# A fused convolution and two-layer kernel on one core: 64-row products of two chunks on the two row halves, g's high part on ScalarE, and a cosine without squaring

## The chip, the core and the metric

The kernel runs on one core of a Trainium2 chip. The core has five engines that run beside each other, each through its own queue in order: TensorE (PE in the profile, its weight loads PEld), VectorE (DVE), ScalarE (ACT), GpSimd (POOL), and SyncE (SP), which issues transfers. They tell each other of finished work by semaphores: an instruction can wait for one and raise one. TensorE multiplies weights of 128 rows with, here, mostly 512 columns of data and adds the results up in PSUM; the data and the weights lie in SBUF. The metric is the time of one execution on the device, in microseconds (us); less is better.

## The reference

```python
# x: 4 x 4096 x 192; weight: 8 x 7
w = softmax(weight)                                       # 7 taps of each of 8 groups of 24 channels
x = causal_conv(x, w).reshape(16384, 192)                 # every channel with the taps of its group
h = x @ moe_w_in;  g = h * np.cos(h);  x = g @ moe_w_out  # 192 -> 2048 -> 192
h = np.maximum(x @ moe2_w_in, 0.0)
out = h * h @ moe2_w_out                                  # 192 -> 2048 -> 192
```

All arrays are f32, and so is the result.

## The kernel before

**Tiles and turns.** The 16384 rows are 32 tiles of 512 tokens; on the chip a tile lies with channels or features in the 128 partitions and tokens along the columns. A *turn* works on four tiles at once: X transposes tile i+1's rows and runs its convolution, A is the first layer (the cosine) of tile i, B the second (the squared relu) of tile i-1, and Y transposes tile i-2's result and stores it. A layer's 2048 features are 16 chunks of 128, taken as 8 *pairs*. Turns -1 to 2 and 31 to 33 are written out; the 28 between are a hardware loop.

**The order within a turn** is a table by hand, `SLOTS`: 18 slots, numbered from 0, as A0 A1 B0 A2 X B1 A3 B2 A4 B3 A5 Y A6 B4 A7 B5 B6 B7. Every engine walks through this table in a `body` of its own, and each does its part of a slot s, or of an earlier one (`turn.earlier(s, n)` is the slot n before s, which at a turn's start is in the turn before). The first tile has another table, `FIRST_SLOTS`.

**Products in parts.** Each operand of a product is kept as a high part rounded to fp32r (`_hi`) and what is left of it (`_lo`). 192 channels are 128 and a *side* of 64. `up(slot)` makes h for the two chunks of a pair; each chunk takes five products of 128 rows: the side's low weights (`up_side_lo`), low weights by high x, high weights by low x, the side's high weights (`up_side_hi`), high by high. The side's x tile, `xin_side`, has its high part in one half of the 128 rows and its low part in the other, and the side's weights stand in both halves. `down(slot)` takes five products of a chunk from `g_hi` and `g_lo` into `y`. TensorE does in slot s `up` of s and then `down` of slot s-3 (`LAG = 3`), if that is an A or a B; so slots 7 and 14, three behind X and Y, have no `down`. h has two buffers in PSUM (`HB = 2`), g and its parts four (`RING = 4`).

**What makes g.** For an A slot: ScalarE reads h into g, scaled by 1/(2 pi) (line 434); VectorE takes the distance to the nearest whole number (`fraction`, lines 529 and 531) into `w`; ScalarE takes the sine of it times pi and squares that (`half_cosine`, lines 444 and 446); VectorE multiplies (`times_cosine`, line 537); GpSimd rounds a copy of g to `g_hi` (line 631); VectorE subtracts that from g for `g_lo` (`low_part`, line 543), for which `down` waits (line 338). For a B slot ScalarE does the relu and the square (lines 436, 438), then GpSimd and VectorE as before. `half_cosine`, `times_cosine`, the copy to `g_hi` and `low_part` are done in slot s for slot s-1; in VectorE's walk `fraction` of s comes first, then `times_cosine`, the taps of the convolution (`TAP_SLOTS`), and `low_part`. At a turn's end stand the splits of x into its parts: the convolution's in slots 15 and 16 (lines 479, 480, 576, 578), layer 1's result in slot 0 (lines 459, 460, and on VectorE `split_layer2`, lines 586 to 594).

**The weights of layer 2** are loaded and split during the first tile, in three rounds in slots 9, 12 and 15 (`LATE_SLOTS`): ScalarE makes the high parts (`late_hi`), GpSimd the low parts (`late_lo_part`) between its copies to `g_hi`, and SyncE then reloads the staging buffer.

## Time and profile before

| | us |
|---|---|
| median of 3 runs | 2639.35 |
| the runs | 2638.49 to 2639.89 |
| profiled execution, first to last instruction | 2636.2 |

A busy share says how long an engine had an instruction in work. TensorE's is modelled: a 512-column product is shown with 0.39 us, yet in a dense stretch the next begins 0.227 us later. So the pace is read from the starts in the timeline, and what an engine waited for from the waits. The turns repeat, so that one of them, here that of 1322 to 1402 us, stands for the loop.

### The profile page before, as it was taken

The numbers are of one execution on the slowest core, as the hardware profiler recorded it, in microseconds if no ns is written. First come the engines' busy times: TensorE is split into PE (matmuls) and PEld (weight loads), VectorE is DVE, ScalarE is ACT, GpSimd is POOL, SyncE is SP. The second block draws the span as 40 slices with busy tenths as digits, with TensorE's granted clock in tenths as the row PEclk, the third lists the DMA queues.
The fourth block names the chain that finished last, engine by engine and source line by source line (L and its number), as shares of the span: only waits on it lengthen the run. The fifth ranks groups of instructions, "written<-read, shape, count | busy, mean of one in ns | idle before, by whom it ended". The sixth has DMA issues, their size and how long they took to land. (4 is left out here: it accounts for less than half of the span.)

```text
span 2636.2 us, 30240 instructions
## 1 busy us (share of the span) xinstructions
PE 2467.1 (94%) x10880; PEld 2003.5 (76%) x10880; DVE 2127.3 (81%) x2060; ACT 1484.8 (56%) x1549; POOL 682.4 (26%) x523
## 2 busy tenths in 40 slices
PE   5799999999999999999999999999999999999998
PEld 4577787777877777777777777778777778777787
DVE  7888888888888887888888888888888888888863
ACT  4455565655555555555555565555656556565554
POOL 2322222222222222222222222222222222222221
PEclk9899999999999999999999999999999999999999
DMA  3100000000000000000000000000000000000000
GB/s 101 36 1 13 13 6 12 12 6 12 12 6 12 6 12 12 12 6 12 6 12 12 6 12 12 6 12 12 6 12 6 12 12 6 12 12 6 6 7 13
DMA packets 39457, 32.89 MB, mean 12 GB/s; under 512 B 1676, under 2 KB 38668, under 8 KB 39180
## 3 DMA queue, kind: packets, MB, share of 16 engines
q1 hardware_dynamic: 39260, 32.61, 4.2%
q8 instruction: 13, 0.21, 0.0%
q14 instruction: 8, 0.07, 0.0%
q10 hardware_dynamic: 176, 0.00, 0.0%
HBM read 20.03 MB, written 12.58 MB: 12 GB/s over the span
## 5 line engine op out<-in xcount | busy, mean ns | idle before, releaser
L631 POOL TENSOR_SCALAR g_hi<-g 128x1024 fp32r<-128x1024 f32 x512 | 658.6, 1297 | 1920.6 <-DVE g L537 1612.2
L543 DVE TENSOR_TENSOR g_lo<-g,g_hi 128x1024 fp32r<-128x1024 f32 x512 | 744.4, 1459 | 167.7 <-POOL g_hi L631 162.0
L444 ACT ACTIVATE w<-w 128x1024 f32<-128x1024 f32 x256 | 271.5, 1061 | 751.2 <-DVE w L531 751.2
L537 DVE SCALAR_TENSOR_TENSOR g<-w,g 128x1024 f32<-128x1024 f32 x256 | 315.7, 1233 | 241.6 <-ACT w L446 239.0
L434 ACT ACTIVATE g<-h 128x1024 f32<-128x1024 f32 x256 | 261.3, 1021 | 268.1 <-PE h L322 268.1
L338 PE MATMUL y_A<-g_hi,dn_lo_A 128*128 128x512 f32 x512 | 222.0, 434 | 125.3 <-DVE g_lo L543 124.6
L531 DVE TENSOR_TENSOR w<-w,g 128x1024 f32<-128x1024 f32 x256 | 313.7, 1225 | 8.8
L436 ACT ACTIVATE g<-h 128x1024 f32<-128x1024 f32 x256 | 259.4, 1013 | 34.8 <-PE h L322 34.6
L438 ACT ACTIVATE g<-g 128x1024 f32<-128x1024 f32 x256 | 271.9, 1062 | 8.1
L446 ACT ACTIVATE w<-w 128x1024 f32<-128x1024 f32 x256 | 271.6, 1061 | 8.1
L570 DVE SCALAR_TENSOR_TENSOR conv_side<-xt_side,taps,conv_side 64x512 f32<-64x512 f32 x192 | 251.3, 1309 | 6.2
L338 PEld LDWEIGHTS y_A<-g_hi,dn_lo_A 128*128 128x128 f32 x512 | 99.1, 194 | 181.8 <-DVE g_lo L543 161.7
L318 PE MATMUL h<-x_side_A,up_side_lo_A 128*128 128x512 f32 x512 | 201.9, 394 | 30.9 <-DVE x_side_A L578 30.9
L529 DVE TENSOR_SCALAR w<-g 128x1024 f32<-128x1024 f32 x256 | 177.8, 695 | 54.0 <-ACT g L434 52.4
L339 PE MATMUL y_A<-g_hi,dn_side_A 128*128 128x512 f32 x512 | 208.2, 407 | 0.0
L340 PE MATMUL y_A<-g_hi,dn_hi_A 128*128 128x512 f32 x512 | 207.8, 406 | 0.0
L341 PE MATMUL y_A<-g_lo,dn_side_A 128*128 128x512 f32 x512 | 206.9, 404 | 0.0
L342 PE MATMUL y_A<-g_lo,dn_hi_A 128*128 128x512 f32 x512 | 206.3, 403 | 0.0
L318 PE MATMUL h<-x_side_B,up_side_lo_B 128*128 128x512 f32 x512 | 201.1, 393 | 2.1 <-ACT g L436 1.1
L338 PE MATMUL y_B<-g_hi,dn_lo_B 128*128 128x512 f32 x512 | 199.6, 390 | 1.4 <-DVE g_lo L543 1.3
L319 PE MATMUL h<-x_hi_B,up_lo_B 128*128 128x512 f32 x512 | 200.5, 392 | 0.0
L320 PE MATMUL h<-x_lo_B,up_hi_B 128*128 128x512 f32 x512 | 200.1, 391 | 0.0
(90 smaller groups left out, 4669.3 us busy)
## 6 DMA issues: line engine op xcount, KB each, us to landing
rows_in<-x SPq DMA_DIRECT2D x32, 384.0 KB, 3.3
out<-late SPq DMA_DIRECT2D x32, 384.0 KB, 2.6
late<-w_out SPq DMA_DIRECT2D x2, 1536.0 KB, 10.2
g<-w_in SPq DMA_DIRECT2D x1, 1024.0 KB, 5.2
g<-w_in SPq DMA_DIRECT2D x2, 512.0 KB, 8.1
late<-w_in SPq DMA_DIRECT2D x2, 512.0 KB, 4.5
late<-w_in SPq DMA_DIRECT2D x4, 256.0 KB, 5.7
taps<-weight ACTq DMA_DIRECT2D x4, 0.7 KB
```

The lines of the kernel that those rows point to most:

```text
L318: pe.matmul(dst, up_side_lo[kind][:, f], xin_side[kind][:, :], start=True, stop=False)
L338: pe.matmul(y[kind][:, 0, :], dn_lo[kind][:, c, :], hi, start=a, stop=False)
L434: act.activation(g[:, r, :, :], src, ACT.Copy, scale=1.0 / TWO_PI).then_inc(taken["A"], 1)
L436: act.activation(g[:, r, :, :], src, ACT.Relu).then_inc(taken["B"], 1)
L438: act.activation(g[:, r, :, :], g[:, r, :, :], ACT.Square).then_inc(relu_sq, 1)
L444: act.activation(v, v, ACT.Sin, scale=math.pi).then_inc(sine, 1)
L446: act.activation(v, v, ACT.Square, scale=math.sqrt(2.0)).then_inc(sine_sq, 1)
L531: dve.tensor_tensor(v, v, u, ALU.subtract).then_inc(frac, 1)
L537: dve.scalar_tensor_tensor(out=u, in0=v, scalar=1.0, in1=u, op0=ALU.subtract, op1=ALU.mult).then_inc(g_made, 1)
L543: dve.tensor_tensor(g_lo[:, r, :, :], g[:, r, :, :], g_hi[:, r, :, :].bitcast(F32), ALU.subtract).then_inc(lo_made[kind], 1)
L570: dve.scalar_tensor_tensor(out=conv_side[side, :], in0=xt_side[side, k:k + TOK], scalar=taps[side, 1, k:k + 1], in1=conv_side[side, :], op ...
L631: return pool.tensor_scalar(dst, src, 1.0, 0.0, ALU.mult, ALU.add)
```

## The change

The products (TensorE). A chunk's `up` has four products of 128 rows: the side's, low by high, high by low, high by high. The side's weights are now one tensor, `up_side`, with the high part in one half of the rows and, in the other, the low part; what is missing, high weights by the side's high x, is one product of 64 rows for each chunk. For the even chunk it is done on the one row half, for the odd chunk on the other, as the last two products of the pair. For this the even chunks' weights stand a second time (`up_even`) and the side's high x a second time (`x_odd`).

g's high part. ScalarE makes it (`high_part`), in slot s for slot s-2, behind its reading of slot s. VectorE's `low_part` is now that of slot s-2 as well. GpSimd's loop is gone; it keeps the low parts of the weights, one behind the other. `LAG` is unchanged.

The cosine. `fraction` rounds u + 1/4 and keeps w = round(u + 1/4) - u; ScalarE takes one sine with a scale and a bias of a quarter turn (`turned_cosine`), always ahead of its reading of the slot; VectorE multiplies, and does so ahead of the next `fraction`.

```diff
-                    pe.matmul(dst, up_side_lo[kind][:, f], xin_side[kind][:, :], start=True, stop=False)
+                    pe.matmul(dst, up_side[kind][:, f], xin_side[kind][:, :], start=True, stop=False)
                     pe.matmul(dst, up_lo[kind][:, f], xin_hi[kind][:, :], start=False, stop=False)
                     pe.matmul(dst, up_hi[kind][:, f], xin_lo[kind][:, :], start=False, stop=False)
-                    pe.matmul(dst, up_side_hi[kind][:, f], xin_side[kind][:, :], start=False, stop=False)
-                    mm = pe.matmul(dst, up_hi[kind][:, f], xin_hi[kind][:, :], start=False, stop=True)
+                    pe.matmul(dst, up_hi[kind][:, f], xin_hi[kind][:, :], start=False, stop=False)
+                even, odd = hi_rows[kind], lo_rows[kind]
+                f = slice((p * PAIR + 1) * P, (p * PAIR + 2) * P)
+                pe.matmul(h[:, s % HB, 0, :], up_even[even, p, :], xin_side[kind][even, :], start=False, stop=True)
+                mm = pe.matmul(h[:, s % HB, 1, :], up_side[kind][odd, f], xin_odd[odd, :], start=False, stop=True)
...
-            def half_cosine(turn, p, back):
+            def turned_cosine(turn, p, back):
                 v = w[:, p % WB, :, :]
                 act.wait_ge(frac, turn.count("A", p, back))
-                act.activation(v, v, ACT.Sin, scale=math.pi).then_inc(sine, 1)
-                act.wait_ge(sine, turn.count("A", p, back))
-                act.activation(v, v, ACT.Square, scale=math.sqrt(2.0)).then_inc(sine_sq, 1)
+                act.activation(v, v, ACT.Sin, bias=quarter[:, 0:1], scale=-TURN).then_inc(cosine, 1)
+
+            def high_part(turn, e, kind, p, back):
+                r = turn.ring(e, back) % RING
+                before = Turn(turn.i - back, TILES, turn.i8 - NP * back)
+                freed = before.before(before.pairs, before.ring(e), RING)
+                if freed:
+                    act.wait_ge(used[freed[0]], freed[1])
+                act.wait_ge({"A": g_made, "B": relu_sq}[kind], turn.count(kind, p, back))
+                act.activation(g_hi[:, r, :, :], g[:, r, :, :], ACT.Copy).then_inc(hi_made[kind], 1)
...
                     if turn.runs(kind):
                         read_h(turn, s, kind, p)
-                    if cosine and kind == "A" and turn.runs("A"):
-                        half_cosine(turn, q, back)
+                    e, back, made, q = turn.earlier(s, 2)
+                    if made in "AB" and turn.runs(made, back):
+                        high_part(turn, e, made, q, back)
...
                         act.activation(xin_side["A"][P - SIDE:P, :], conv_side[P - SIDE:P, :], ACT.Copy)
+                        act.activation(xin_odd[0:SIDE, :], conv_side[P - SIDE:P, :], ACT.Copy)
...
-                dve.tensor_scalar(v, u, ROUND, ROUND, ALU.add, ALU.subtract).then_inc(whole, 1)
+                dve.tensor_scalar(v, u, 0.25, ROUND, ALU.add, ALU.add).then_inc(whole, 1)
                 dve.wait_ge(whole, turn.count("A", p))
-                dve.tensor_tensor(v, v, u, ALU.subtract).then_inc(frac, 1)
+                dve.scalar_tensor_tensor(out=v, in0=v, scalar=ROUND, in1=u, op0=ALU.subtract,
+                                         op1=ALU.subtract).then_inc(frac, 1)
...
+                dve.tensor_copy(xin_odd[SIDE:P, :], y_side[low, :])
                 dve.tensor_copy(xin_side["B"][low, :], y_side[low, :]).then_inc(x2_step, 1)
...
+                    if last == "A" and turn.runs("A", back):
+                        times_cosine(turn, r, q, back)
                     if kind == "A" and turn.runs("A"):
                         fraction(turn, turn.ring(s) % RING, p)
-                    if last == "A" and turn.runs("A", back):
-                        times_cosine(turn, r, q, back)
...
-                    if last in "AB" and turn.runs(last, back):
-                        low_part(turn, r, last, q, back)
+                    e, back, made, q = turn.earlier(s, 2)
+                    if made in "AB" and turn.runs(made, back):
+                        low_part(turn, turn.ring(e, back) % RING, made, q, back)
```

Where the instructions stand. On TensorE the `up` of one pair, A, before:

```order
L318 MATMUL h<-x_side_A,up_side_lo_A 128x512
L319 MATMUL h<-x_hi_A,up_lo_A 128x512
L320 MATMUL h<-x_lo_A,up_hi_A 128x512
L321 MATMUL h<-x_side_A,up_side_hi_A 128x512
L322 MATMUL h<-x_hi_A,up_hi_A 128x512
L318 MATMUL h<-x_side_A,up_side_lo_A 128x512
L319 MATMUL h<-x_hi_A,up_lo_A 128x512
L320 MATMUL h<-x_lo_A,up_hi_A 128x512
L321 MATMUL h<-x_side_A,up_side_hi_A 128x512
L322 MATMUL h<-x_hi_A,up_hi_A 128x512
```

and after:

```order
L330 MATMUL h<-x_side_A,up_side_A 128x512
L331 MATMUL h<-x_hi_A,up_lo_A 128x512
L332 MATMUL h<-x_lo_A,up_hi_A 128x512
L333 MATMUL h<-x_hi_A,up_hi_A 128x512
L330 MATMUL h<-x_side_A,up_side_A 128x512
L331 MATMUL h<-x_hi_A,up_lo_A 128x512
L332 MATMUL h<-x_lo_A,up_hi_A 128x512
L333 MATMUL h<-x_hi_A,up_hi_A 128x512
L336 MATMUL h<-x_side_A,up_even 128x512
L337 MATMUL h<-x_odd,up_side_A 128x512
```

Still ten products; the last two, lines 336 and 337, are those on half the rows.

On ScalarE, in the loop, slots 7 and 8 (B2 and A4), before; line 434 and 436 read an A and a B, `w<-w` is the sine and its square, `g<-g` the relu's square:

```order
L444 ACTIVATE w<-w 128x1024
L446 ACTIVATE w<-w 128x1024
L414 REGISTER_ALU
L436 ACTIVATE g<-h 128x1024
L438 ACTIVATE g<-g 128x1024
L414 REGISTER_ALU
L434 ACTIVATE g<-h 128x1024
```

and after, where line 456 reads B2, line 454 A4, and line 474 is the copy to `g_hi`:

```order
L464 ACTIVATE w<-w,quarter 128x1024
L434 REGISTER_ALU
L456 ACTIVATE g<-h 128x1024
L458 ACTIVATE g<-g 128x1024
L474 ACTIVATE g_hi<-g 128x1024
L434 REGISTER_ALU
L454 ACTIVATE g<-h 128x1024
L474 ACTIVATE g_hi<-g 128x1024
```

The squared sine is gone, and behind each reading stands the copy of the pair two slots back.

On VectorE, in the loop, slots 8 and 9 (A4 and B3), before; lines 529 and 531 are the fraction of A4, 537 the product with the cosine, 568 and 570 a tap of the convolution:

```order
L529 TENSOR_SCALAR w<-g 128x1024
L531 TENSOR_TENSOR w<-w,g 128x1024
L542 REGISTER_ALU
L543 TENSOR_TENSOR g_lo<-g,g_hi 128x1024
L537 SCALAR_TENSOR_TENSOR g<-w,g 128x1024
L567 REGISTER_ALU
L568 SCALAR_TENSOR_TENSOR conv<-xt,taps,conv 128x512
L570 SCALAR_TENSOR_TENSOR conv_side<-xt_side,taps,conv_side 64x512
L543 TENSOR_TENSOR g_lo<-g,g_hi 128x1024
```

and after:

```order
L559 TENSOR_SCALAR w<-g 128x1024
L561 SCALAR_TENSOR_TENSOR w<-w,g 128x1024
L573 TENSOR_TENSOR g_lo<-g,g_hi 128x1024
L568 TENSOR_TENSOR g<-w,g 128x1024
L597 REGISTER_ALU
L598 SCALAR_TENSOR_TENSOR conv<-xt,taps,conv 128x512
L600 SCALAR_TENSOR_TENSOR conv_side<-xt_side,taps,conv_side 64x512
L572 REGISTER_ALU
L573 TENSOR_TENSOR g_lo<-g,g_hi 128x1024
```

The rows have the same order, but the first `g_lo` is that of A3 after the change, where it was B2's before, and the second that of B2, where it was A4's.

## Rows read from the trace of the kernel before

**Rows 1.** The page, part 1: each engine's busy us, share of the span, instructions.
```profile
PE 2467.1 (94%) x10880; PEld 2003.5 (76%) x10880; DVE 2127.3 (81%) x2060; ACT 1484.8 (56%) x1549; POOL 682.4 (26%) x523
```

**Rows 2.** The waits: who waited for whom, us in total, times, longest.
```profile
DVE g L537 <- ACT w L446: 239.0, 188, 2.2
...
PEld y_A L338 <- DVE g_lo L543: 161.7, 114, 6.8
```

**Rows 3.** The edge copy, line 552: times, ns min/median/max, first and last start.
```profile
L552 DVEq FUSED_REGOPS  x28: 75/75/75, 285.0 to 2451.9; - x28
```

**Rows 4.** Timeline: start us, us, engine line op, tile; TensorE, `up` to `down`.
```profile
1326.54 0.39 PE L322 MATMUL h<-x_hi_B,up_hi_B 128*128 128x512 f32 x1
1326.77 0.39 PE L338 MATMUL y_B<-g_hi,dn_lo_B 128*128 128x512 f32 x1
```

**Rows 5.** Timeline, weight loads of X's transposes.
```profile
1321.33 0.14 PEld L354 LDWEIGHTS h<-ident,rows_in 128*128 128x128 f32 x1
1321.44 0.14 PEld L353 LDWEIGHTS h<-ident,rows_in 128*128 128x128 f32 x1
```

**Rows 6.** Timeline, TensorE and VectorE around a wait; brackets: idle before, and releaser.
```profile
1368.21 0.39 PE L322 MATMUL h<-x_hi_B,up_hi_B 128*128 128x512 f32 x1
1368.48 1.95 DVE L543 TENSOR_TENSOR g_lo<-g,g_hi 128x1024 fp32r<-128x1024 f32 x1
...
1370.48 0.50 PE L338 MATMUL y_A<-g_hi,dn_lo_A 128*128 128x512 f32 x1 [1.89 <-DVE g_lo L543]
...
1370.82 0.40 PE L339 MATMUL y_A<-g_hi,dn_side_A 128*128 128x512 f32 x1
```

**Rows 7.** Timeline, ScalarE: a B slot's pair, and two copies in the first tile.
```profile
45.76 1.04 ACT L403 ACTIVATE up_hi_B<-late 128x1024 fp32r<-128x1024 f32 x1
46.71 1.04 ACT L404 ACTIVATE up_side_hi_B<-late 128x1024 fp32r<-128x1024 f32 x1
...
1326.97 1.03 ACT L436 ACTIVATE g<-h 128x1024 f32<-128x1024 f32 x1 [0.26 <-PE h L322]
1328.03 1.06 ACT L438 ACTIVATE g<-g 128x1024 f32<-128x1024 f32 x1
```

**Rows 8.** Timeline, an A slot's reading on ScalarE and VectorE behind it; two VectorE steps.
```profile
1334.17 1.23 DVE L531 TENSOR_TENSOR w<-w,g 128x1024 f32<-128x1024 f32 x1
1335.32 1.22 DVE L543 TENSOR_TENSOR g_lo<-g,g_hi 128x1024 fp32r<-128x1024 f32 x1
...
1390.30 1.03 ACT L434 ACTIVATE g<-h 128x1024 f32<-128x1024 f32 x1 [3.58 <-PE h L322]
1391.36 0.69 DVE L529 TENSOR_SCALAR w<-g 128x1024 f32<-128x1024 f32 x1 [1.47 <-ACT g L434]
1392.09 1.23 DVE L531 TENSOR_TENSOR w<-w,g 128x1024 f32<-128x1024 f32 x1
```

**Rows 9.** Timeline, VectorE at a turn's start: y's split, then A0's fraction.
```profile
1384.20 0.68 DVE L586 TENSOR_TENSOR y_side<-y_A,y_side 64x512 f32<-64x512 f32 x1
1384.91 0.57 DVE L589 CAST x_side_B<-y_side 64x512 fp32r<-64x512 f32 x1
1385.40 0.67 DVE L591 TENSOR_TENSOR x_lo_B<-y_A,x_hi_B 128x512 fp32r<-128x512 f32 x1
1386.09 0.69 DVE L594 TENSOR_TENSOR x_side_B<-y_side,x_side_B 64x512 fp32r<-64x512 f32 x1
1386.80 0.69 DVE L529 TENSOR_SCALAR w<-g 128x1024 f32<-128x1024 f32 x1
```

**Rows 10.** Line 543, `g_lo`: times, ns min/median/max, first and last start.
```profile
L543 DVE TENSOR_TENSOR g_lo<-g,g_hi x512: 1210/1225/3382, 40.6 to 2625.9; 128x1024 fp32r<-128x1024 f32 x171
```

**Rows 11.** Busy us by engine in 8 us; behind POOL's the granted clock.
```profile
1448.00:1456.00 8.00, 6.15 (x20) 4.58 (x20) 6.85 (x7) 3.60 (x5) 1.43 (x2) 0.79 0.00 0
```

**Rows 12.** Timeline, ScalarE: the first tile's first reading of A, and the next's.
```profile
31.25 1.03 ACT L434 ACTIVATE g<-h 128x1024 f32<-128x1024 f32 x1 [6.62 <-PE h L322]
...
101.95 1.03 ACT L434 ACTIVATE g<-h 128x1024 f32<-128x1024 f32 x1 [1.08 <-PE h L322]
```

More of the change, by code:

```diff
@@ L59 @@
 ROUND = 1.5 * 2.0 ** 23
+TURN = 13176794.0 * 2.0 ** -21
+QUARTER = 13176794.0 * 2.0 ** -23
 def at(t):
@@ L162, in tile_program @@
         xin_side = {k: sb(f"x_side_{k}", [P, TOK], F32R) for k in "AB"}
+        xin_odd = sb("x_odd", [P, TOK], F32R)
+        low, high = slice(0, SIDE), slice(SIDE, P)
+        hi_rows, lo_rows = {"A": high, "B": low}, {"A": low, "B": high}
         g = sb("g", [P, RING, PAIR, TOK])
@@ L207, in tile_program @@
         taken = {k: sem(f"taken_{k}") for k in "ABXY"}
-        sine = sem("sine")
-        sine_sq = sem("sine_sq")
+        cosine = sem("cosine")
         relu_sq = sem("relu_sq")
@@ L281, in _ @@
                 sp.wait_ge(late_lo, 2 * half + 2)
+                if half:
+                    sp.wait_ge(even_made, half)
                 cols = slice(half * HALF, (half + 1) * HALF)
@@ L450, in body @@
                     _, back, last, q = turn.earlier(s, 1)
-                    cosine = last == "A" and turn.runs("A", back)
-                    if cosine and not (kind == "A" and turn.runs("A")):
-                        half_cosine(turn, q, back)
+                    if last == "A" and turn.runs("A", back):
+                        turned_cosine(turn, q, back)
                     if s == 0 and turn.runs("A", 1):
@@ L603, in body @@
                         split_layer2(turn)
+                    if last == "A" and turn.runs("A", back):
+                        times_cosine(turn, r, q, back)
                     if kind == "A" and turn.runs("A"):
                         fraction(turn, turn.ring(s) % RING, p)
-                    if last == "A" and turn.runs("A", back):
-                        times_cosine(turn, r, q, back)
                     if turn.runs("X") and s == taps_at[0]:
@@ L647, in _ @@
             pool.wait_ge(wi_hi, 1)
-            pool.tensor_tensor(up_side_lo["A"][:, :], stage_in[:, F:2 * F],
-                               up_side_hi["A"][:, :].bitcast(F32), ALU.subtract).then_inc(wi_lo, 1)
-            def body(turn):
-                for s, (kind, p) in enumerate(turn.slots()):
-                    e, back, last, q = turn.earlier(s, 1)
-                    if last in "AB" and turn.runs(last, back):
-                        r = turn.ring(e, back) % RING
-                        before = Turn(turn.i - back, TILES, turn.i8 - NP * back)
-                        freed = before.before(before.pairs, before.ring(e), RING)
-                        if freed:
-                            pool.wait_ge(used[freed[0]], freed[1])
-                        made = {"A": g_made, "B": relu_sq}[last]
-                        pool.wait_ge(made, turn.count(last, q, back))
-                        round_hi(g_hi[:, r, :, :], g[:, r, :, :]).then_inc(hi_made[last], 1)
-                    if turn.peeled and turn.i == 0 and s in LATE_SLOTS:
-                        late_lo_part(1 + LATE_SLOTS.index(s))
-            turns(pool, body)
+            split = up_side["A"][hi_rows["A"], :]
+            pool.tensor_tensor(split, stage_in[hi_rows["A"], F:2 * F], split.bitcast(F32),
+                               ALU.subtract).then_inc(wi_lo, 1)
+            for n in range(1, 1 + len(LATE_SLOTS)):
+                late_lo_part(n)
 def kernel(x, weight, moe_w_in, moe_w_out, moe2_w_in, moe2_w_out):
```

41 lines of the change are left out of this document (23 added, 18 removed).

## The prediction

> **What bounds the kernel now.** The first view is busy time by engine [rows 1]: TensorE (PE) 94%, VectorE 81%, ScalarE 56%, GpSimd 26%. The reader would take TensorE for the bound. The list of waits corrects that [rows 2]: TensorE's largest wait is for `g_lo`, VectorE's last step of a pair, 161.7 us in 114 times; and VectorE itself waits 239.0 us for ScalarE's square. Next, how long is a turn (18 slots, 16 pairs)? The conv's edge copy stands once in a turn; in the loop it stands 28 times, from 285.0 to 2451.9 us, so a turn takes 80.26 us [rows 3]. Then the pace of TensorE: one 512-column product starts 0.227 us after the other [rows 4]. A pair has 20 of them, 4.53 us; 16 pairs are 72.5 us; X and Y I put at 0.9 and 1.0 us, from 0.11 for each of their transposes [rows 5], so 74.4 us are streams and 5.8 us of each turn are waits. One of them is in the timeline [rows 6]: the `up` of a slot is out at 1368.44, `g_lo` ends at 1370.43, TensorE goes on at 1370.48. So at several places of a turn VectorE sets the end; a prediction needs the chain of hand-overs, not the sum of products.
>
> **Part 1, fewer product times.** The side's high part of two chunks is now one product on the lower and one on the upper 64 rows. If the two run beside each other, `up` has 9 product times instead of 10: 2.04 us instead of 2.27, a slot (U + D = `up` + `down`) 4.31 instead of 4.53. No row has a product on half the rows. The lower end of the two's cost is 0.227, since each streams 512 columns and the row has that pace; nothing can be gained below it. The upper end is 2 x 0.227 = 0.454, one after the other. I take 0.227, for the weights need not hold it up: loads for the transposes follow each other in 0.11 us [rows 5], two in 0.22. Saved by itself: 16 x 0.227 = 3.6 us a turn, 109 us in 30 turns.
>
> The Trainium skill is of two minds here. "TensorE: Matmul & The Clock Gate", Part 3, has products on different row groups run concurrently; that agrees with the lower end, and no row here shows it. "TensorEngine Tiling (Array Packing)", Key Properties, says that changing the tiling mode drains TensorE, and each pair would change it twice. That speaks against this change, is a rival below, and no row shows it either.
>
> **Part 2, GpSimd's copy goes to ScalarE, one slot later.** Gone are 512 GpSimd copies. With them goes a slowing of VectorE: `g_lo` has a median of 1225 ns but a longest of 3382 ns [rows 10], and 1.95 us where the copy ran beside it [rows 6]. That is relief on VectorE, hidden wherever the next part decides. Added on ScalarE are 512 copies SBUF to SBUF, 1.04 us each, 0.95 apart from the next [rows 7]; removed are 256 squares of about the same length. ScalarE was busy 1484.8 / 32 = 46.4 us a tile [rows 1]; it gets 16 x 1.04 and loses 8 x 1.06, so some 55 of 80 us, below the bound as a sum. But its order matters. The copy of pair s-2 stands behind the reading of slot s, which waits for `up` of slot s. VectorE's `g_lo` of s-2 stands behind the fraction of slot s, which waits for that reading too. And `down` of s-2 is the `down` of slot s+1, since LAG is still 3. Before, `g_lo` of s-1 was made in slot s, and nothing tied these.
>
> So there is a new chain. Let f be the end of the stream of `up` in slot s, and L the time from f to the `down` that it lets go:
> - A slot: ScalarE starts 0.20 after f [rows 4, 7], reads 1.03, hand-over 0.03, the rounding and its hand-over 0.73, then the second step, behind which `g_lo` starts 1.15 later and takes 1.22 [rows 8], then 0.05 to TensorE [rows 6]. L_A = 4.41.
> - B slot: 0.20, relu to square 1.06, square to copy 0.95, copy 1.04 [rows 7], 0.03, `g_lo` 1.22, 0.05. L_B = 4.55.
> After a pause the first product takes 0.34 instead of 0.227 to the next [rows 6]: 0.11 more. So from one `down` start d to that two slots on, an A slot between them gives 4.31 + 4.41 + 0.11 = 8.83, a B slot 8.97, against 8.62 of pure products where both slots are whole. It bites most where a slot has little for TensorE: X and Y (about 1 us instead of `up`) and slots 7 and 14, which have no `down` (their pair three slots back is X or Y). In slot 8 TensorE has only 2.04 us of `up` after slot 7's, but `down` must wait 4.55: a pause of 2.5 us where there was none.
>
> **Part 3, the turn's end.** The conv split has one more 64x512 copy on ScalarE (under the 1.04 of the wide one; I take 0.6), y's split one more on VectorE (0.49). VectorE does slot 17's `g_lo`, then y's split, then A0's fraction, and only then the `g_lo` of slot 16, wanted in slot 1. From f17: 0.20+1.06+0.95+1.04+0.03 = 3.28 to `g_lo`, 1.15 to y's split, 0.71+0.49+0.49+0.69+0.71 for it, where the 0.49 stands twice for the added copy [rows 9], 0.73+1.15 for the fraction, 1.22 and 0.05, 0.11 restart: 10.78. ScalarE's extra copy is covered by slot 16's `up`, for whose end the next reading waits; the cover is thin, and without it the copy costs its 0.6.
>
> **Part 4, the cosine.** One sine with a bias instead of sine and square: on ScalarE 1.06 us less of a pair; on VectorE the same three steps in other forms, so nothing. The 1.09 us that VectorE idled for the square are gone, but they lay in the old chain. `times_cosine` now stands before the next fraction; the sine ends 4.3 us after f, just when slot s+1's `up` is out, so it hides.
>
> **The sum of a turn.** Take the longest way through the 18 slots from `down` of slot 15 to the next one: two plain slots and the end of the turn (4.31+4.31+10.78 = 19.40) to slot 1; plain, 4.31, to slot 2; through A in slot 3, 8.83, to 4; through B in 5, 8.97, to 6; through B in 7, 8.97, to 8; plain, 4.31, to 9; through A in 10, 12 and 14, 3 x 8.83, to 15. Sum 81.28 us. Of this TensorE's U + D stands in it ten times, so the saving counts 10 x 0.227 and not 16 x.
>
> To it comes the clock. Behind a pause of about 1.9 us the granted clock fell in some turns: 0.79 over 8 us in one turn [rows 11], the lower of the levels 1.2 and 2.4 GHz for a part of it, after TensorE had paused; 8 x 0.21 = 1.7 us of TensorE's time. Now two pauses a turn have about 2.5 us and one 1.8. I take one fall a turn, a third of it on the path: 0.5 us (ends 0 and 3.4). A turn: 81.8 against 80.26, +1.5 us.
>
> **The whole.** 30 turns x 1.5 = +46 us. The first tile: from the first reading of A to the next tile's took 70.7 us [rows 12], because GpSimd had the late weights' low parts and the copies in one queue; now the copies leave that queue, and about 57 us remain (VectorE 4.2 us a pair and the taps, then the last weights' load), while the start has two more copies on ScalarE, some 1.7 us: -12 us (ends -20 and +3). The last tile, products alone: -2 us. So 2636.2 + 46 - 12 - 2 = 2668; outside the span lie 2639.35 - 2636.2 = 3.2 us, so 2671 us against the median of 2639.35, 1.2% slower. An error of 0.1 us in each of the seven hand-overs would be 0.7 us a turn, 21 us.
>
> **The rivals.**
> - Faster: the hand-overs have more slack than I give them (readings or `g_lo` start earlier in the turn than the walk says), and TensorE's stream decides. Then each turn has 16 x 4.31 + 1.9 = 70.9 us and pauses like the old 5.8: 76.7, 3.6 less, 2639 - 107 = 2530; half of that 2585. For it: VectorE's relief is large. Against: the queues' order is fixed, and L rests on rows. It decides from where L falls below 4.2. Chance 0.20.
> - The halves don't overlap (the change doesn't do what it says): 0.454 a pair of products, 10 x 0.227 = 2.27 a turn, +68: 2739. Chance 0.12.
> - Each switch between whole and half rows empties the array. A product shows 0.39 us but paces 0.227 [rows 4], so emptying costs 0.16, twice a pair 0.33; 10 x 0.33 x 30 = +99: 2770. Chance 0.08. (This is the Tiling page's rule above; without that page the price stands.)
> - The clock falls at both long pauses and all of it is on the path: 3.4 instead of 0.5 a turn, +87: 2758. Chance 0.10.
>
> **How the numbers follow.** The forecast, 2671 with its own range of 2640 to 2705, has 0.50. A difference of 0.2%, 5 us, is what a measurement can tell: below 2634 lies the faster rival and a small part of the forecast's lower side, 0.22; within it 0.05; above 0.73. The range goes down to 2560, which takes the nearer half of the faster rival, and up to 2762; left out are the other half (0.10) and the emptying array (0.08).
>
> **What would show it.** In the changed kernel's trace: a turn of 81 to 82 us by the edge copy; waits of TensorE for `g_lo` of both A and B, in sum 9 to 11 us a turn; pauses of about 2.4 us in slots 8 and 15 and 1.7 in slot 1; the two half products starting within some 0.02 us of each other, or else 0.227 apart; `g_lo` near 1.22 in all cases, no 1.95. The forecast is wrong if TensorE's sum of waits stays at 5 us a turn, or if a slot's `g_lo` is made well before `up` of the slot behind it is out.

## The result

| | before | after |
|---|---|---|
| median of the runs on the same chip, us | 2639.11 | 2889.8 |
| the runs, us | 2638.49 to 2639.89 | 2887.75 to 2892.18 |
| profiled execution, us | 2636.2 | 2887.7 |
| a turn by the edge copy, us | 80.26 | 87.12 |
| mean granted clock | 0.985 | 0.963 |

The changed kernel is slower: the ratio of the times is 1.095, interval 1.0935 to 1.0966. The sign was forecast; the size was not, and 2889.8 us lies outside the range of 2560 to 2762.

The page's first part, against [rows 1]:

```profile
PE 2615.2 (91%) x10880; PEld 1921.7 (67%) x10880; DVE 1881.8 (65%) x2093; ACT 1772.4 (61%) x1840; POOL 25.1 (1%) x11
```

The waits (who waited for whom: us in total, times, longest), against [rows 2]:

```profile
PEld h L336 <- issue: 181.0, 512, 0.7
PEld y_A L353 <- DVE g_lo L573: 171.6, 189, 6.3
PEld y_B L353 <- DVE g_lo L573: 142.1, 122, 4.7
...
DVE g L568 <- ACT w L464: 42.7, 35, 1.2
```

The edge copy, now line 582, against [rows 3]:

```profile
L582 DVEq FUSED_REGOPS  x28: 75/75/75, 298.9 to 2651.1; - x28
```

TensorE has 10880 products as before, but 2615 busy us instead of 2467. Its waits for VectorE are now for `g_lo` of A and of B, 171.6 + 142.1 us. VectorE's wait for ScalarE's cosine fell from 239.0 to 42.7 us, and GpSimd is idle: what the change wanted of these two engines it got. A new wait is TensorE's largest, that of the first half product's weights for "issue" (time in which the profile shows nothing that it waited for), once in each of the 512 `up`s. A turn takes (2651.1 - 298.9) / 27 = 87.12 us.

**Where the 251.5 us of the span went.** The 27 turns between the first and the last edge copy: 27 x 6.86 = 185.2. Before the first edge copy: 298.9 - 285.0 = 13.9. Behind the last one: 236.6 instead of 184.3, so 52.3. The two ends together are a quarter of the loss.

**The pair of half products.** TensorE in the timeline of the changed kernel, the end of an `up` of an A and the start of the `down` behind it (start us, us, engine line op, tile, rows*columns of the weights, rows x columns of the data):

```profile
1438.44 0.39 PE L333 MATMUL h<-x_hi_A,up_hi_A 128*128 128x512 f32 x1
1438.76 0.49 PE L336 MATMUL h<-x_side_A,up_even 64*128 64x512 f32 x1
...
1438.76 0.49 PE L337 MATMUL h<-x_odd,up_side_A 64*128 64x512 f32 x1
...
1439.18 0.50 PE L353 MATMUL y_A<-g_hi,dn_lo_A 128*128 128x512 f32 x1
...
1439.52 0.40 PE L354 MATMUL y_A<-g_hi,dn_side_A 128*128 128x512 f32 x1
```

The two halves (lines 336 and 337, `64*128`) start at the same moment. But the first starts 0.32 us behind the whole product ahead of it, the next whole product 0.42 behind them, and the one after that 0.34, where 0.227 is the pace [rows 4]. Beyond one product that is 0.09 + 0.20 + 0.11 = 0.40 us. The pair of halves costs 0.63, two whole products cost 0.454: the change made `up` longer, and a slot takes 4.73 us instead of 4.53. (Of these 0.20 us 0.18 are in the distances just named; the products right behind are a few ns further apart too.)

**The chain of hand-overs.** The same turn from the end of slot 7's `up` to slot 8's `down`, on all engines; in brackets the idle time before an instruction and what ended it:

```profile
1443.48 0.50 PE L337 MATMUL h<-x_odd,up_side_B 64*128 64x512 f32 x1
...
1444.03 1.03 ACT L456 ACTIVATE g<-h 128x1024 f32<-128x1024 f32 x1 [0.53 <-PE h L337]
...
1445.08 1.06 ACT L458 ACTIVATE g<-g 128x1024 f32<-128x1024 f32 x1
...
1446.05 1.04 ACT L474 ACTIVATE g_hi<-g 128x1024 fp32r<-128x1024 f32 x1
...
1447.12 1.23 DVE L573 TENSOR_TENSOR g_lo<-g,g_hi 128x1024 fp32r<-128x1024 f32 x1 [0.93 <-ACT g_hi L474]
...
1448.40 0.50 PE L353 MATMUL y_B<-g_hi,dn_lo_B 128*128 128x512 f32 x1 [1.95 <-DVE g_lo L573]
```

`up` of slot 7 (a B), reading, square, copy to `g_hi`, `g_lo`, `down`: each waits for the one above it, and TensorE stands still for 1.95 us although slot 8's `up` was long out. It is the chain of Part 2, link by link: from the start of the reading, at 1444.03, to the `down` it takes 4.37 us, where the prediction had 1.06 + 0.95 + 1.04 + 0.03 + 1.22 + 0.05 = 4.35. From the `down` of slot 6, at 1439.18, to that of slot 8, at 1448.40, it is 9.22 us, for which the walk had 8.97.

**The clock.** Busy us by engine in stretches of 4 us around this pause; behind POOL's the granted clock:

```profile
1444.00:1448.00 4.00, 2.45 (x10) 1.52 (x10) 3.04 (x4) 3.94 (x5) 0.00 (x0) 1.00 0.00 0
1448.00:1452.00 4.00, 3.60 (x10) 2.84 (x11) 3.88 (x5) 2.10 (x2) 0.00 (x0) 0.67 0.00 0
1452.00:1456.00 4.00, 4.00 (x16) 2.81 (x15) 2.07 (x3) 1.08 (x2) 0.00 (x0) 0.90 0.00 0
```

The granted clock is full ahead of the pause, and then 0.67 and 0.90 in the next two stretches: TensorE ran at the lower of its two levels for a part of them, with 0.43 us between products. The pause in slot 15 of this turn (1.78 us) is followed by a stretch at 0.64. From the `down` of slot 8 to that of 9 it took 6.38 us, from 15 to 16 6.34, where a plain slot takes 4.73 to 4.78: 1.6 us each, and nothing lay beside it. Not every turn has both: of the 54 pauses in slots 8 and 15 of the 27 turns, 41 were followed by such a long slot, 2.4 us a turn in the mean.

### The profile page after: what moved, and what is told of

It is laid out like the page before. It is cut to its first block, busy times and chain, and to the rows that moved or that the text cites. A ratio compares the mean times of both kernels' runs of the same rounds, so it can differ in the third digit from the quotient of the medians.

```text
span 2887.7 us, 29490 instructions
## 1 busy us (share of the span) xinstructions
PE 2615.2 (91%) x10880; PEld 1921.7 (67%) x10880; DVE 1881.8 (65%) x2093; ACT 1772.4 (61%) x1840; POOL 25.1 (1%) x11
## 4 chain that ended last, share of the span: by engine, by line
PE 66%; DVE 18%; ACT 9%; issue 5%; DMA 0%; ACTq 0%; DVEq 0%; SPq 0%
DVE g_lo L573 7%; PE h L330 6%; PE h L331 6%; PE h L332 6%; PE h L333 6%; PE h L336 6%; PE y_A L353 5%; PE y_B L353 5%; DVE w L561 4%; ACT g L454 3%; PE y_B L356 3%; PE y_B L357 3%; PE y_B L355 3%; PE y_B L354 3%; PE y_A L357 3%
## 5 line engine op out<-in xcount | busy, mean ns | idle before, releaser
L573 DVE TENSOR_TENSOR g_lo<-g,g_hi 128x1024 fp32r<-128x1024 f32 x512 | 630.4, 1232 | 582.5 <-ACT g_hi L474 581.4
L474 ACT ACTIVATE g_hi<-g 128x1024 fp32r<-128x1024 f32 x512 | 535.6, 1047 | 0.8
L464 ACT ACTIVATE w<-w,quarter 128x1024 f32<-128x1024 f32 x256 | 294.5, 1150 | 368.9 <-DVE w L561 368.9
L568 DVE TENSOR_TENSOR g<-w,g 128x1024 f32<-128x1024 f32 x256 | 318.1, 1243 | 60.4 <-ACT w L464 42.7
L561 DVE SCALAR_TENSOR_TENSOR w<-w,g 128x1024 f32<-128x1024 f32 x256 | 313.7, 1225 | 8.8
L353 PEld LDWEIGHTS y_A<-g_hi,dn_lo_A 128*128 128x128 f32 x512 | 100.4, 196 | 205.4 <-DVE g_lo L573 171.6
L330 PE MATMUL h<-x_side_A,up_side_A 128*128 128x512 f32 x512 | 204.5, 399 | 21.7 <-DVE x_side_A L608 21.2
L353 PEld LDWEIGHTS y_B<-g_hi,dn_lo_B 128*128 128x128 f32 x512 | 98.7, 193 | 187.6 <-DVE g_lo L573 142.1
L330 PE MATMUL h<-x_side_B,up_side_B 128*128 128x512 f32 x512 | 210.3, 411 | 1.1 <-ACT g L456 1.1
L357 PE MATMUL y_B<-g_lo,dn_hi_B 128*128 128x512 f32 x512 | 210.1, 410 | 0.0
L356 PE MATMUL y_B<-g_lo,dn_side_B 128*128 128x512 f32 x512 | 210.0, 410 | 0.0
L355 PE MATMUL y_B<-g_hi,dn_hi_B 128*128 128x512 f32 x512 | 209.0, 408 | 0.0
```

The source lines that it names most:

```text
L330: pe.matmul(dst, up_side[kind][:, f], xin_side[kind][:, :], start=True, stop=False)
L353: pe.matmul(y[kind][:, 0, :], dn_lo[kind][:, c, :], hi, start=a, stop=False)
L355: pe.matmul(y[kind][:, 0, :], dn_hi[kind][:, c, :], hi, start=False, stop=False)
L356: pe.matmul(y[kind][:, 1, :], dn_side[kind][:, c, :], lo, start=False, stop=z)
L357: mm = pe.matmul(y[kind][:, 0, :], dn_hi[kind][:, c, :], lo, start=False, stop=z)
L464: act.activation(v, v, ACT.Sin, bias=quarter[:, 0:1], scale=-TURN).then_inc(cosine, 1)
```

## The experiments

The first question is what the loss is made of: the half rows, the copy's new place, or both.

**Nine whole products.** The changed kernel with one whole product in place of the two halves.

```diff
-                    pe.matmul(dst, up_hi[kind][:, f], xin_hi[kind][:, :], start=False, stop=False)
...
-                pe.matmul(h[:, s % HB, 0, :], up_even[even, p, :], xin_side[kind][even, :], start=False, stop=True)
-                mm = pe.matmul(h[:, s % HB, 1, :], up_side[kind][odd, f], xin_odd[odd, :], start=False, stop=True)
+                    pe.matmul(dst, up_hi[kind][:, f], xin_hi[kind][:, :], start=False, stop=n == 0)
+                mm = pe.matmul(dst, up_side[kind][:, f], xin_side[kind][:, :], start=False, stop=True)
```

> The changed kernel, but the two 64-row products of a pair are one product of 128 rows, into the odd chunk only (so the side's high by high is left out and something else added in its place: the output is not the reference's). `up` is nine products in one mode, which is just what the prediction had assumed of the pair of halves. Theory 1 (the price is the change between whole and half rows, 0.40 us a pair beyond one product's 0.227): a slot falls from 4.73 to 4.31 us, the turn from 87.1 to 81.3 us of the prediction's walk, plus up to 3.4 us of lower clock, so 2655 to 2755 us. Rival (the price lies in ScalarE's and VectorE's order alone, TensorE's products don't matter): 2860 us or more.

Measured: 2728.59 us, ratio 1.0346 (1.0329 to 1.0364), clock 0.984. Its edge copy:

```profile
L579 DVEq FUSED_REGOPS  x28: 75/75/75, 291.1 to 2504.6; - x28
```

A turn is (2504.6 - 291.1) / 27 = 81.98 us. This kernel has just the TensorE work that the prediction assumed, 19 whole product times for `up` and `down` of a pair, and its turn is the one that the walk gave, 81.8. The parts of the walk agree too (means over the 27 turns): from the `down` of slot 15 to that of slot 1 19.28 us (walk 19.40), from 6 to 8 9.04 (8.97), from 13 to 15 8.88 (8.83). So the walk over the hand-overs was right, and what a turn lost beyond it, 87.12 - 81.98 = 5.14 us, 161 us in all, is the price of the half rows.

That price has two terms. The long slots behind a pause are 9 here, in 54 pauses of 2.38 and 2.20 us, 0.5 us a turn; in the changed kernel they are 41, 2.4 us. So 1.9 of the 5.14 us are the clock, and 3.2 the longer `up`.

**Both halves on the same row half.** Do the halves overlap at all?

```diff
-                mm = pe.matmul(h[:, s % HB, 1, :], up_side[kind][odd, f], xin_odd[odd, :], start=False, stop=True)
+                mm = pe.matmul(h[:, s % HB, 1, :], up_even[even, p, :], xin_side[kind][even, :], start=False, stop=True)
```

> The changed kernel, but both 64-row products of a pair are on the same row half (the odd chunk gets the even chunk's product: the output is not the reference's). The two can't run beside each other. Theory 1 (halves overlap, the changes of mode cost on top): the second starts 0.227 us behind the first instead of 0.01, the other distances stay (0.31 before, 0.42 behind), the slot is 4.95 us and the kernel 2950 to 3000 us. Rival (the 0.42 behind the pair is the second product's own time, not a change of mode): no change, 2890 us.

Measured: 2941.37 us (one execution), a turn of 88.76; a little under the expected band. TensorE's timeline:

```profile
1405.38 0.50 PE L336 MATMUL h<-x_side_A,up_even 64*128 64x512 f32 x1
1405.72 0.39 PE L337 MATMUL h<-x_side_A,up_even 64*128 64x512 f32 x1
1406.05 0.50 PE L353 MATMUL y_B<-g_hi,dn_lo_B 128*128 128x512 f32 x1
```

Now the second half starts 0.34 behind the first. In the changed kernel they start together, so the overlap is real and belongs to the two row halves. It is worth 1.6 us a turn here. The expectation had 0.227 between the halves and 0.42 behind them; it is 0.34 and 0.33. So a half product that follows another on the same half, with no change between whole and half rows, costs 0.11 beyond the pace as well, and the 0.42 belongs to the two that run together. How the 0.40 us of the pair divides between the change and the half products themselves, these runs don't separate: each has one way in and one way out for each pair.

**The half rows alone**, in the kernel before. g's high part, the cosine and the order stay.

```diff
-                    pe.matmul(dst, up_side_hi[kind][:, f], xin_side[kind][:, :], start=False, stop=False)
-                    mm = pe.matmul(dst, up_hi[kind][:, f], xin_hi[kind][:, :], start=False, stop=True)
+                    pe.matmul(dst, up_hi[kind][:, f], xin_hi[kind][:, :], start=False, stop=False)
...
+                pe.matmul(h[:, s % HB, 0, :], up_even[even, p, :], xin_side[kind][even, :], start=False, stop=True)
+                mm = pe.matmul(h[:, s % HB, 1, :], up_side[kind][odd, f], xin_odd[odd, :], start=False, stop=True)
```

> The kernel before with the half-row products alone: GpSimd's copy, the squared cosine and every order as before. Theory 1: a slot has 4.71 instead of 4.53 us of products, 16 x 0.18 = 2.9 us a turn, of which part disappears in the 5.8 us of waits that a turn has: 2650 to 2735 us, most likely 2690. Rival (the half-row products gain, and all the loss is from the other parts): below 2630 us.

Measured: 2621.6 us, ratio 0.9939 (0.9923 to 0.9956), clock 0.993. A miss for both theories: 0.6% *faster*, small but clear of the noise. From here on the views say why. Its edge copy gives (2432.5 - 285.4) / 27 = 79.52 us a turn. Its wait for the cosine is what it was, and TensorE's for `g_lo` of A has fallen from 161.7 us:

```profile
L569 DVEq FUSED_REGOPS  x28: 75/75/75, 285.4 to 2432.5; - x28
```

```profile
DVE g L554 <- ACT w L462: 238.9, 188, 2.2
...
PEld y_A L349 <- DVE g_lo L560: 82.8, 77, 6.5
```

So TensorE's longer pair is covered. Its plain slots do take 4.73 instead of 4.53 us, but in the turn of 1322 to 1402 us it paused once for VectorE, 1.38 us, where it had paused 1.16, 1.89 and 0.62 before: VectorE, with its wait for ScalarE's square, still sets when the turn goes on, and the longer slots fill the pauses. The gain of 0.74 us a turn has the size of one other thing, the conv's last subtraction. It is line 578 in the kernel before, and line 595 here (times, ns min/median/max), first the kernel before, then this one:

```profile
L578 DVE TENSOR_TENSOR x_side_A<-conv_side,x_side_A x32: 686/1436/1441, 26.0 to 2505.2; 64x512 fp32r<-64x512 f32 x32
```

```profile
L595 DVE TENSOR_TENSOR x_side_A<-conv_side,x_side_A x32: 686/687/690, 26.3 to 2486.0; 64x512 fp32r<-64x512 f32 x32
```

1436 ns became 687. The extra copy on ScalarE moved it away from GpSimd's copy to `g_hi`, as I read the timeline. VectorE's own next step is no earlier for it: it now waits 0.95 us for `g_hi` in each turn. What is earlier is the next turn's first `up`, which reads this result: within the 27 turns TensorE's wait for it falls from 16.7 to 6.5 us. That this is the whole 0.74 is argued from the sizes alone; the trace has another difference, no fall of the clock in slot 15, where the kernel before has 11 in 27 turns.

**Part 1 undone.** The changed kernel with five whole products of a chunk again.

```diff
-                    pe.matmul(dst, up_hi[kind][:, f], xin_hi[kind][:, :], start=False, stop=False)
...
-                pe.matmul(h[:, s % HB, 0, :], up_even[even, p, :], xin_side[kind][even, :], start=False, stop=True)
-                mm = pe.matmul(h[:, s % HB, 1, :], up_side[kind][odd, f], xin_odd[odd, :], start=False, stop=True)
+                    pe.matmul(dst, up_side_hi[kind][:, f], xin_side[kind][:, :], start=False, stop=False)
+                    mm = pe.matmul(dst, up_hi[kind][:, f], xin_hi[kind][:, :], start=False, stop=True)
```

> The changed kernel with its half-row products undone: ten whole products in `up` as before; ScalarE's copy, the later g_lo and the cosine stay. Theory 1 with the prediction's walk: U + D is 4.53, the walk gives 81.3 + 10 x 0.227 = 83.5 us a turn, plus up to 3.4 us of lower clock: 2720 to 2825 us. It is faster than the changed kernel by 0.18 x 10 to 16 a turn, 50 to 90 us at least. Rival (all the loss is the half rows'): 2640 us or less.

Measured: 2802.89 us, ratio 1.0627 (1.0609 to 1.0644), clock 0.977, a turn of 84.21. The half rows, with the two small copies that they need at the turn's end, cost the changed kernel 87 us; the other 164 us of the loss come with the rest of the change.

**The parts first.** The rest has three pieces: the copy on ScalarE, its place behind the reading of the slot, and the cosine. Here the work stays on its engines, but the high and the low part of pair s-2 are made ahead of slot s's reading and fraction, first with the half rows, then with whole rows.

```diff
                 for s, (kind, p) in enumerate(turn.slots()):
+                    e, back, made, q = turn.earlier(s, 2)
+                    if made in "AB" and turn.runs(made, back):
+                        high_part(turn, e, made, q, back)
                     _, back, last, q = turn.earlier(s, 1)
                     if last == "A" and turn.runs("A", back):
                         turned_cosine(turn, q, back)
...
                     if turn.runs(kind):
                         read_h(turn, s, kind, p)
-                    e, back, made, q = turn.earlier(s, 2)
-                    if made in "AB" and turn.runs(made, back):
-                        high_part(turn, e, made, q, back)
```

and so on VectorE for `low_part`.

> The changed kernel with one order changed: in each slot ScalarE makes the high part and VectorE the low part of the pair two slots back ahead of the slot's own reading and fraction, so neither waits for this slot's `up` any more. Half-row products stay. Theory (the chain of hand-overs costs the waits): TensorE's products decide, 16 x 4.71 + 1.9 = 77.3 us a turn and 1 to 2 us at the turn's end, clock nearly whole: 2540 to 2600 us. Rival (waits come from VectorE's or ScalarE's amount of work): little changes, 2850 us or more.

> The same order, and the half-row products undone (ten whole products): 16 x 4.53 + 1.9 = 74.4 us a turn and 1 to 2 us at its end: 2450 to 2520 us, faster than both kernels. If the half rows' price is as read (0.18 us a pair against two whole products), it is 16 x 0.18 x 30 = 87 us faster than the run with half rows. Rival (something else of the copy on ScalarE costs): above 2560 us.

Measured: with half rows 2574.53 us, ratio 0.9757 (0.9741 to 0.9773), a turn of 77.88; with whole rows 2471.83, ratio 0.9372 (0.9356 to 0.9388), a turn of 74.69. Two findings. The same copies on the same engine, moved ahead of a reading and of a fraction, are worth 2803 - 2472 = 331 us with whole rows, and 2890 - 2575 = 315 us with half rows: their place made the loss, not their time. Which of the two moves, ScalarE's or VectorE's, counts for more was not tried. And the half rows cost 102.7 us here, 0.20 us in each of 512 pairs: the 4.73 against 4.53 of a slot, with no cover left; 87 had been expected, from 0.18. The waits of the kernel with half rows:

```profile
PEld y_B L353 <- issue: 61.1, 249, 1.5
PEld y_A L353 <- issue: 46.4, 187, 1.2
PEld y_A L353 <- DVE g_lo L573: 27.9, 8, 9.6
```

The wait for `g_lo` of A, 171.6 us after the change, is 27.9.

**The cosine alone**, in the kernel before: old order, GpSimd's copy, whole rows. VectorE's fraction and product have the change's forms too.

```diff
-                act.activation(v, v, ACT.Sin, scale=math.pi).then_inc(sine, 1)
-                act.wait_ge(sine, turn.count("A", p, back))
-                act.activation(v, v, ACT.Square, scale=math.sqrt(2.0)).then_inc(sine_sq, 1)
+                act.activation(v, v, ACT.Sin, bias=quarter[:, 0:1], scale=-TURN).then_inc(sine_sq, 1)
```

> The kernel before with the cosine without squaring alone, all orders as they were. ScalarE's chain is 1.06 us shorter, and VectorE waited 1.09 us for it in most A slots. Theory (VectorE with that pause was late in the old kernel): a pair of slots falls from 9.4 to TensorE's 9.07 us, 2 to 4 us a turn, 2520 to 2580 us. Rival (the pause was hidden): 2635 us.

Measured: 2468.8 us, ratio 0.9354 (0.9338 to 0.937), 51 us below the expected band: the gain was undersized even here. It is the fastest kernel of this study that does the whole work. Its page, waits and edge copy:

```profile
PE 2409.9 (98%) x10880; PEld 1994.4 (81%) x10880; DVE 2120.5 (86%) x2061; ACT 1260.7 (51%) x1293; POOL 673.7 (27%) x523
```

```profile
DVE g L539 <- ACT w L446: 38.3, 32, 1.2
...
PEld y_A L340 <- DVE g_lo L544: 26.5, 11, 6.6
```

```profile
L553 DVEq FUSED_REGOPS  x28: 75/75/75, 271.0 to 2287.5; - x28
```

VectorE's wait for the cosine fell from 239.0 to 38.3 us, and TensorE's for `g_lo` of A from 161.7 to 26.5; VectorE's busy time, 2120.5 us against 2127.3, is nearly what it was, so its new forms are not the gain. A turn is 74.69 us; the prediction's streams without any wait were 74.4. TensorE is busy 98% of the span: here it is the bound, and there is nothing left for the other parts of the change to gain by freeing engines.

**The cosine with the half rows.** If TensorE is the bound in the kernel above, the half rows must cost it their full price, though they had cost the kernel before nothing. On top of the cosine's edit:

```diff
-                    mm = pe.matmul(dst, up_hi[kind][:, f], xin_hi[kind][:, :], start=False, stop=True)
+                    pe.matmul(dst, up_hi[kind][:, f], xin_hi[kind][:, :], start=False, stop=False)
...
+                pe.matmul(h[:, s % HB, 0, :], up_even[even, p, :], xin_side[kind][even, :], start=False, stop=True)
+                mm = pe.matmul(h[:, s % HB, 1, :], up_side[kind][odd, f], xin_odd[odd, :], start=False, stop=True)
```

> The kernel before with the cosine without squaring and the half-row products; GpSimd keeps its copy. With the new cosine TensorE alone sets the turn (74.7 us), so the half rows' price is no longer hidden: 16 x 0.20 = 3.2 us a turn more, 2565 to 2580 us, although the same edit without the new cosine made the kernel 16 us faster. Rival (half rows gain here too): below 2469 us.

Measured: 2568.28 us, ratio 0.9733 (0.9717 to 0.9749), a turn of (2379.4 - 276.7) / 27 = 77.88. That is 3.19 us a turn above 74.69, 16 x 0.20, and 99.5 us in all. The cover was the pauses that came with the wait for the square.

**The halves at the head of `up`.** Is it their place at the end, ahead of `down`, that is dear?

```diff
+                pe.matmul(h[:, s % HB, 0, :], up_even[even, p, :], xin_side[kind][even, :], start=True, stop=False)
+                pe.matmul(h[:, s % HB, 1, :], up_side[kind][odd, f], xin_odd[odd, :], start=True, stop=False)
                 for n in range(PAIR):
...
```

> The changed kernel with the two 64-row products at the head of `up` instead of its end. Theory 1 (each change between whole and half rows costs by itself, wherever it stands): 0.3 us into the pair, 0.4 out of it, the slot stays at 4.7 us, 2870 to 2910 us. Rival (part of the price is the wait for g_lo or the weights of `down` behind the pair): the slot is 4.5 us or less, below 2830 us.

Measured: 2919.61 us (one execution), a turn of 88.01, 10 us above the expected band. TensorE's timeline:

```profile
1414.57 0.39 PE L357 MATMUL y_B<-g_lo,dn_hi_B 128*128 128x512 f32 x1
1414.89 0.50 PE L329 MATMUL h<-x_side_B,up_even 64*128 64x512 f32 x1
...
1415.32 0.50 PE L334 MATMUL h<-x_side_B,up_side_B 128*128 128x512 f32 x1
1415.65 0.39 PE L335 MATMUL h<-x_hi_B,up_lo_B 128*128 128x512 f32 x1
```

The same 0.32, 0.43 and 0.33. The price goes with the half rows and not with their place or with the `down` behind them.

**The copy and the order alone.** The changed kernel with whole rows and with the squared sine again (VectorE's old fraction and product with it).

```diff
-                act.activation(v, v, ACT.Sin, bias=quarter[:, 0:1], scale=-TURN).then_inc(cosine, 1)
+                act.activation(v, v, ACT.Sin, scale=math.pi).then_inc(sine, 1)
+                act.wait_ge(sine, turn.count("A", p, back))
+                act.activation(v, v, ACT.Square, scale=math.sqrt(2.0)).then_inc(cosine, 1)
```

> The changed kernel with whole rows in `up` and with the squared cosine of before: what is left of the change is GpSimd's copy on ScalarE and the order that goes with it. Theory (hand-overs): the sine and its square end 5.4 us after f, later than the next slot's `up` (4.53 + 0.2), so each reading behind an A slot is 0.6 us later than in the run with whole rows and the new cosine; on the turn's longest way this stands three to six times: 2 to 4 us a turn, 2860 to 2930 us. Rival (waits of other places cover it): 2803 us as with the new cosine.

Measured: 2904.89 us, ratio 1.1006 (1.0988 to 1.1024), clock 0.959, a turn of 87.57. The copy in its new place and the order that goes with it cost 267 us, and the new cosine gives 102 of them back (2905 to 2803).

**Nine products and the parts first.** What would a pair of halves that cost one product be worth, in the better order? The parts first, and of `up`:

```diff
...
-                pe.matmul(h[:, s % HB, 0, :], up_even[even, p, :], xin_side[kind][even, :], start=False, stop=True)
-                mm = pe.matmul(h[:, s % HB, 1, :], up_side[kind][odd, f], xin_odd[odd, :], start=False, stop=True)
+                mm = pe.matmul(dst, up_side[kind][:, f], xin_side[kind][:, :], start=False, stop=True)
```

> Nine whole products in `up` as in the first experiment (output not the reference's: the side's high by high is left out) and both parts of g ahead of the slot's reading: what the change would give if the pair of halves cost one product's time and the hand-overs were out of the way. 16 x 4.31 + 1.9 + 0.3 = 71.2 us a turn, 2350 to 2385 us. Rival (VectorE, ScalarE or the clock become the bound): above 2420 us.

Measured: 2410.35 us (one execution), a turn of 72.70, some 25 us above the expected band: from the `down` of slot 16 to that of 17 and of slot 0 to that of 1 it takes 4.97 and 4.98 instead of 4.31 (TensorE waits 0.52 and 0.50 us for `g_lo`), and four other slots are 0.11 to 0.15 longer. Against 2471.83 with whole rows, ten products against nine, it is 61 us: so much the halves could bring if a pair of them cost one product's time.

| kernel | us | a turn | against before |
|---|---|---|---|
| before | 2639 | 80.26 | 1 |
| + half rows | 2622 | 79.52 | 0.994 |
| + cosine | 2469 | 74.69 | 0.935 |
| + cosine, half rows | 2568 | 77.88 | 0.973 |
| + copy and order | 2905 | 87.57 | 1.101 |
| + copy, order, cosine | 2803 | 84.21 | 1.063 |
| + copy, order, cosine, half rows (the change) | 2890 | 87.12 | 1.095 |
| the change, parts first | 2575 | 77.88 | 0.976 |
| the change, parts first, whole rows | 2472 | 74.69 | 0.937 |

## Why the prediction was right in sign and wrong in size

**Right: the chain of hand-overs.** The order on two queues, read before the change ran, gave a turn of 81.8 us; with the TensorE work that the walk assumed it is 81.98. The long pauses stood where the walk put them, in slots 8 and 15 (1.95 and 1.78 us; 2.38 and 2.20 with nine whole products, where the prediction had about 2.4), and `g_lo` is 1225 ns in the median as before, but 1232 instead of 1459 in the mean, now without GpSimd's copies beside it. The reason given for "slower" is shown: with the parts first the same work takes 315 us less.

**Where the 219 us beyond 2671 lie.** The kernel with nine whole products takes 2729 us, 57 above 2671, and its turn is right to 0.2 us: those 57 are the two ends, put at -14 us and measured at +42. The other 161 us came with the half rows.

**The term that failed: the pair of half products**, put at 0.227, ends 0.227 and 0.454. It is 0.63, above both ends. The overlap was forecast rightly. The step that failed is the bound's: "one after the other" was taken as the worst, as if a product's start depended on its own stream alone. Going to half rows and back costs 0.40 us on top of the stream. Yet it doesn't stand in the turn ten times in full, as U + D does in the walk: that would be 4.0 us, and 3.2 were measured. Where TensorE pauses behind `up`, the late starts behind the pair fall into the pause: from the `down` of slot 6 to that of 8 it is 9.22 us against 9.04, only 0.18 more. The rest of the 5.14 us is the clock. The rival "each switch empties the array" had the nearest mechanism and nearly the price, 0.33, with a chance of 0.08, and 2770 us was left out of the range. The Trainium skill says so outright ("TensorEngine Tiling (Array Packing)", Key Properties: changing the mode drains TensorE), and the trace agrees in kind, 0.32 and 0.42 around the pair; "TensorE: Matmul & The Clock Gate", Part 3 (row groups run concurrently) agrees too, with starts 0.00 to 0.01 us apart. The two rules do not contradict each other: both hold, and the prediction weighed them as if one had to fall.

**The clock**, 0.5 us a turn. In the turn shown the granted clock fell behind both long pauses, and each fall cost 1.6 us on the path, 3.3 together: the rival's 3.4. In the mean of 27 turns it is 2.4. With nine whole products it is the forecast's 0.5, though the pauses there are longer; that was one whole fall in every third turn and not a third of one in each, so the agreement is luck. What made the clock fall so much more often with the half rows stays open. Behind a pause on the critical chain the engine that resumes is the bound at that moment, so nothing covers it.

**The last tile, -2 us: wrong in sign.** Behind the last edge copy it is 52.3 us more, and still 35.9 more with nine whole products (220.2 against 184.3). The step that failed: in the last turns only B's slots run, and the prediction took "products alone" and left the chain out, where it bites hardest. The changed kernel's timeline there:

```profile
2823.92 0.50 PE L337 MATMUL h<-x_odd,up_side_B 64*128 64x512 f32 x1
...
2824.46 1.02 ACT L456 ACTIVATE g<-h 128x1024 f32<-128x1024 f32 x1 [3.84 <-PE h L337]
...
2825.51 1.06 ACT L458 ACTIVATE g<-g 128x1024 f32<-128x1024 f32 x1
...
2826.47 1.04 ACT L474 ACTIVATE g_hi<-g 128x1024 fp32r<-128x1024 f32 x1
...
2827.55 1.23 DVE L573 TENSOR_TENSOR g_lo<-g,g_hi 128x1024 fp32r<-128x1024 f32 x1 [8.07 <-ACT g_hi L474]
...
2828.83 0.80 PE L353 MATMUL y_B<-g_hi,dn_lo_B 128*128 128x512 f32 x1 [4.41 <-DVE g_lo L573]
```

Between `up` and `down` of the slot there is nothing else for TensorE: 4.41 us idle, then products at the lower clock (0.80 us shown instead of 0.39 to 0.50). The `down`s of these pairs start 9.2 to 10.6 us apart; before, neighbours there were mostly 4.5 to 5.0 apart.

**The first tile, -12 us: wrong.** From the first reading of A to the next tile's it took 72.0 us, not 57 or 58; before it was 70.7 [rows 12]. GpSimd's queue was said to hold the late weights up. With its copies gone, its last low part of the second round did end earlier, at 69.5 instead of 76.7 us, but the tile was no shorter: TensorE's longest wait there is in both kernels for the conv's last subtraction on VectorE, 21.2 us and before 20.5. What would shorten that wasn't tried.

**The cosine, "nothing": right for this sum, wrong as a reading of the kernel before.** "They lay in the old chain" should have been priced: in the old order this part alone takes 170 us off, the largest single gain, and in the new order 102. It was VectorE's largest wait [rows 2], 239.0 us. The prediction walked the new order only. A walk of the old one, where sine and square stand between a fraction and its product, might have named the square. It might also have foretold that the half rows alone cost nothing in the kernel before, which both theories of that experiment missed.

**Small.** The sine with a bias from a [128, 1] tile takes longer than the one without, and the prediction had them alike. Line 464 on the page (busy us, mean ns):

```profile
L464 ACT ACTIVATE w<-w,quarter 128x1024 f32<-128x1024 f32 x256 | 294.5, 1150 | 368.9 <-DVE w L561 368.9
```

1150 ns instead of 1060. It costs nothing here, since it hides as forecast.

## What to carry to other kernels

When work moves to another engine's queue, ask what it now stands behind: a lagged step placed behind the current slot's reading inherits that reading's wait, and the place of one copy and one subtraction was worth 331 us of 2803 here. Walk each part of a composed change alone on the *old* order too, and start with the largest wait of the engine that the busiest one waits for (here VectorE's for the square; GpSimd and ScalarE have larger waits, both for VectorE). Its removal was the whole gain that this change had in it (0.935), and the other two parts spent it. A saving counted in products must include the products around it whose start it delays.

## What the runs showed of the hardware

- Two 64-row products of 512 columns on the two row halves start together (0.00 to 0.01 us apart); on the same half the second starts 0.34 behind the first.
- Going from whole rows to a pair of half products and back costs 0.40 us beyond one product: 0.32, then 0.42 and 0.34 between starts, where 0.227 is the pace, at the head of `up` as at its end. With both on the same half it is 0.32, 0.34, 0.33 and 0.34. The half product's weight load waits each time, 181.0 us in 512 times, instead of going ahead under the product before it.
- A 64x512 subtraction on VectorE took 1436 ns in the median in the kernel before, with some 0.9 us of GpSimd's copy beside it, and 687 in the one with the half rows alone, with some 0.3 us of it, and in the changed kernel, with none.
- In the turn shown, pauses of TensorE of 1.95 and 1.78 us on the chain were each followed by a stretch with a granted clock of 0.67 and 0.64 of full speed. Over 27 turns this came behind 41 of 54 such pauses; with nine whole products, behind 9 of 54 pauses of 2.38 and 2.20 us. So the length of the pause alone doesn't tell it.
